# Attention inputs laid out by channel: no transposes in, one scan for the states, 96-column sums on TensorE

## The reference, cut to what matters

```python
for t in range(S):                                   # S = 768
    kt, vt, rt, wt = (k[:, :, t], v[:, :, t], r[:, :, t], w[:, :, t])
    cur = np.einsum('bhd,bhe->bhde', u[None] * kt, vt)
    y[:, :, t] = np.einsum('bhd,bhde->bhe', rt, state + cur)
    state = wt[:, :, :, None] * state + np.einsum('bhd,bhe->bhde', kt, vt)
x = _moe_ref(x=x, **moe_kwargs)      # dense: every token through 8 experts
return _moe2_ref(x=x, **moe2_kwargs) # routed: every token through one expert
```

## Time and profile before

| | |
|---|---|
| time, median of 3 runs | 1204.25 us (1198.97 to 1204.97) |
| time of the profiled execution | 1201.32 us |
| its span | 1199.6 us |
| PE busy in the span | 97% |
| DVE, ACT, POOL busy | 42%, 37%, 20% |
| last instruction of the attention ends | 150.34 us |
| mean granted clock of TensorE, whole span | 0.978 |
| mean granted clock, 25.30 to 138.60 us | 0.80 |

### The profile page before, as it was taken

How to read it: one execution, slowest core, us unless ns; L and a number is a source line. 1 busy time by engine, 2 the same in 40 slices (tenths; PEclk the granted TensorE clock), 3 DMA queues, 4 the chain that set the end, 5 groups by cost and what they waited for, 6 DMA issues and landing times. The chain is left out here.

```text
span 1199.6 us, 18556 instructions
## 1 busy us (share of the span) xinstructions
PE 1161.1 (97%) x6968; PEld 1039.6 (87%) x6968; DVE 504.4 (42%) x949; ACT 448.9 (37%) x926; POOL 243.8 (20%) x247
## 2 busy tenths in 40 slices
PE   6999989999999999999999999999999998999997
PEld 4888769899999998999999899999999986999997
DVE  5777556222222222212222222212222353999996
ACT  4565352212212211221221122122123473888884
POOL 5544262202201210220221121022012210000001
PEclk9888799999999999999999999999999999999999
DMA  9741043040050031005005002200300303999991
GB/s 187 144 70 31 2 149 124 26 160 1 1 186 1 1 132 55 1 2 185 1 1 185 1 1 91 94 1 1 105 1 1 132 35 114 392 358 368 359 361 59
DMA packets 106982, 123.41 MB, mean 103 GB/s; under 512 B 52745, under 2 KB 95406, under 8 KB 106912
## 3 DMA queue, kind: packets, MB, share of 16 engines
q1 hardware_dynamic: 104928, 117.65, 31.1%
q0 software_dynamic: 1984, 4.75, 1.0%
HBM read 98.37 MB, written 25.39 MB: 103 GB/s over the span
## 5 line engine op out<-in xcount | busy, mean ns | idle before, releaser
L973 DVE SCALAR_TENSOR_TENSOR h_lo<-hid,h_hi 128x512 fp32r<-128x512 f32 x168 | 116.1, 691 | 497.8 <-ACT h_hi L836 497.8
L836 ACT ACTIVATE h_hi<-hid 128x512 fp32r<-128x512 f32 x168 | 100.5, 598 | 547.7 <-PE hid L1131 547.7
L794 POOL TENSOR_TENSOR w_lo<-raw,w_hi 128x384 fp32r<-128x384 f32 x128 | 130.8, 1022 | 644.2 <-ACT w_hi L828 644.2
L1144 PE MATMUL acc<-w_hi,h_hi 128*128 128x384 f32 x736 | 249.6, 339 | 0.0
L1144 PE MATMUL acc<-w_hi,h_lo 128*128 128x384 f32 x736 | 249.3, 339 | 0.0
L1144 PE MATMUL acc<-w_lo,h_hi 128*128 128x384 f32 x736 | 248.6, 338 | 0.0
L1131 PE MATMUL hid<-x_hi,w_hi 128*128 128x512 f32 x576 | 227.9, 396 | 0.5 <-issue 0.4
L1131 PE MATMUL hid<-x_hi,w_lo 128*128 128x512 f32 x576 | 227.6, 395 | 0.0
L1131 PE MATMUL hid<-x_lo,w_hi 128*128 128x512 f32 x576 | 227.3, 395 | 0.0
L1144 PEld LDWEIGHTS acc<-w_lo,h_hi 128*128 128x128 f32 x736 | 138.1, 188 | 8.6
L1144 PEld LDWEIGHTS acc<-w_hi,h_hi 128*128 128x128 f32 x736 | 138.1, 188 | 7.7
(11 more groups left out here) (255 smaller groups left out, 1464.1 us busy)
## 6 DMA issues: line engine op xcount, KB each, us to landing
raw<-in_moe_w SPq DMA_DIRECT2D x54, 1536.0 KB, 9.2
rows<-filler SPq DMA_DIRECT2D x8, 2328.0 KB, 16.4
m_x<-rows SPq DMA_DIRECT2D x19, 194.0 KB, 4.6
spread_w<-in_w SPq DMA_DIRECT2D x16, 144.0 KB, 4.2
spread_r<-in_r SPq DMA_DIRECT2D x16, 144.0 KB, 4.1
spread_k<-in_k SPq DMA_DIRECT2D x16, 144.0 KB, 4.3
v_sb<-in_v SPq DMA_DIRECT2D x16, 144.0 KB, 4.2
out_y<-m_y,m_token POOLq DMA_INDIRECT x19, 6.7
```

Of the source, the lines that this page charges most:

```text
L794: pool.tensor_tensor(lo[q][m][:, a:b], raw[m][:, a:b], hi[q][m][:, a:b].bitcast(F32), ALU.subtract).then_inc(s_wlo, 1)
L836: act.activation(h_hi[st % HB][:, :], hid[st % HB][:, :], ACT.Relu).then_inc(s_hhi, 1)
L973: dve.scalar_tensor_tensor(h_lo[st % HB][:, :], hid[st % HB][:, :], 0.0, h_hi[st % HB][:, :].bitcast(F32), ALU.max, ALU.subtract).then_inc ...
L1144: mm = pe.matmul(acc[j][:, 0:DM], a[st % HB][:, j * P:(j + 1) * P], b[q][1][:, f * DM:(f + 1) * DM], start=(f == 0 and x == 0), stop=(f == ...
```

## The change

The host lays the inputs out before the launch. `laid_out` gives r and k by channel, with 64 rows for each head and zeros in rows 48 to 63, w in the same way with ones there and with the scan's zeros between the blocks, v by token and padded to one run per partition, and u as 96 columns for each pair of heads, of which two hold u and the other 94 are zero. So each of a pair's inputs is one DMA, straight into `w_pad`, `k_ch`, `r_ch` and `v_sb`, and `turn_in`, `channels`, the `spread` tensors and their memsets go.

The u term is now one POOL multiplication of 768 columns (`rk`), six PE matmuls of 96 columns (`sums`), and a copy of 12 columns on ACT (`current`). The states are one DVE scan over 240 columns with a table `carry`, which ACT fills (`carries`). Scores have four PSUM banks in place of two. On DVE both scans of the next pair are ahead of the states of this one. `keep_clock` has one matmul of 240 columns for each pair, where it had three of 256 (`FIRST, BACK, LAST = 5, 1, 4`: five ahead of the first pair, one for each later pair, four at the end).

```diff
@@ sync
-                for n in "wrk":
-                    for h in two:
-                        sp.dma_start(spread[n][q][:, :, h, 0:D], src[n][i, h]).then_inc(s_in[n][q], 16)
+                load(w_pad, w, "w", i)
+                load(k_ch, k, "k", i)
+                load(r_ch, r, "r", i)
@@ gpsimd
-                pool.tensor_tensor(rku[:, :, :, :], spread["r"][q][:, :, :, 0:D], spread["k"][q][:, :, :, 0:D], ALU.mult).then_inc(s_rk, 1)
-                pool.tensor_tensor(rku[:, :, :, :].rearrange("p n h d -> p n (h d)"), rku[:, :, :, :].rearrange("p n h d -> p n (h d)"),
-                                   u_rows[:, c:c + 2 * D].unsqueeze(1).broadcast_to([P, NT, 2 * D]), ALU.mult).then_inc(s_rku, 1)
+                if j >= 1:
+                    pool.wait_ge(s_sums, j)
+                pool.tensor_tensor(rk[:, :], r_ch[j % 2][:, :], k_ch[j % 2][:, :], ALU.mult).then_inc(s_rk, 1)
+            receiver_keys(0)
+            for j in range(PAIRS):
+                scaled(j)
+                if j + 1 < PAIRS:
+                    receiver_keys(j + 1)
+                current_values(j)
@@ scalar
-                act.activation(block_w[q][:, :, 1:BLK1], turn_a[:, 0:S].rearrange("p (n c) -> p n c", c=BLK), ACT.Copy).then_inc(s_chan["w"], 1)
-                act.activation(r_ch[q][:, :], turn_b[:, 0:S], ACT.Copy).then_inc(s_chan["r"], 1)
-                act.activation(k_ch[q][:, :], turn_a[:, 0:S], ACT.Copy).then_inc(s_chan["k"], 1)
+            def carries(j):
...
+                act.activation(carry[j % 2][:, :, 1:NT - 1], coef_r[:, 1:NT - 1, BT].unsqueeze(1).broadcast_to([P, D, NT - 2]),
+                               ACT.Copy).then_inc(s_carry, 1)
+            def current(j):
+                act.wait_ge(s_sums, j + 1)
...
+                act.activation(flat(cur[j % 2][:, :, :]), turn[:, CUR:CUR + NT * 2], ACT.Copy).then_inc(s_cur, 1)
+            current(0)
+            for j in range(PAIRS):
+                divided(j, 0)
+                carries(j)
+                rows(j)
+                halves(j)
+                divided(j, 1)
+                diagonal(j)
+                if j + 1 < PAIRS:
+                    current(j + 1)
@@ vector
-                dve.tensor_copy(st[:, 1, :], inc[:, 0, :]).then_inc(s_step, 1)
-                for t in range(1, NT - 1):
-                    dve.wait_ge(s_step, (NT - 2) * i + t)
-                    step = dve.scalar_tensor_tensor(st[:, t + 1, :], st[:, t, :], coef_r[:, t, BT:BT + 1], inc[:, t, :], ALU.mult, ALU.add)
-                dve.tensor_reduce(cur[:, :, :], rku[:, :, :, :], AX.X, ALU.add).then_inc(s_cur, 1)
+                dve.tensor_tensor_scan(state[q][:, :, :].rearrange("p d t -> p (d t)"), carry[q][:, :, :].rearrange("p d t -> p (d t)"),
+                                       turn[:, 0:(NT - 1) * D], 0.0, ALU.mult, ALU.add).then_inc(s_state, 1)
             for i in range(-1, PAIRS):
+                if ahead:
+                    before_block(i + 1)
+                if ahead:
+                    behind_block(i + 1)
                 if back:
                     states(i)
-                if ahead:
-                    before_block(i + 1)
+                if i >= 1:
+                    outputs(i - 1, 1)
@@ tensor
+            def sums(j):
+                pe.wait_ge(s_rk, j + 1)
+                for t in range(NT):
+                    mm = pe.matmul(turn[:, CUR + 2 * t:CUR + 2 * t + WIDE], rk[:, t * P:(t + 1) * P], u_cols[:, j % (H // 2), :],
+                                   start=True, stop=True, skip_group_check=True)
+                mm.then_inc(s_sums, 1)
+            for j in range(PAIRS):
+                pe.wait_ge(s_cur, j + 1)
+                keep_clock(FIRST if j == 0 else BACK)
+                turn_back(j)
+                if j >= 1:
+                    out_tiles(j - 1, 1)
+                increments(j)
+                scores(j, 0)
+                if j + 1 < PAIRS:
+                    sums(j + 1)
+                scores(j, 1)
+                out_tiles(j, 0)
```

More of the change, by code:

```diff
@@ L89, in attention @@
         k_rows = sb("k_rows", [P, NT, P])
[L90 removed]
+        state = [sb(f"state{q}", [P, D, NT - 1]) for q in two]
         state_diag = [sb(f"state_diag{q}", [P, NT, 2, 64]) for q in two]
[L92 to L93 removed]
+        carry = [sb(f"carry{q}", [P, D, NT - 1]) for q in two]
+        rk = sb("rk", [P, S])
+        cur = [sb(f"cur{q}", [P, NT, 2]) for q in two]
         cur_v = sb("cur_v", [P, NT, 2, D])
         scores_sb = [[sb(f"scores_sb{g}{h}", [P, TG, P]) for h in two] for g in range(G)]
[L97 to L99 removed]
+        turn = ps("turn", [P, 1024])
+        CUR, IDLE = S, S + 16
+        score = [[ps(f"score{g}{h}", [P, 512]) for h in two] for g in range(G)]
         yps = [ps(f"yps{g}", [P, 512]) for g in range(G)]
@@ L297, in _ @@
             dve.memset(tile_end[:, :, BT:BT1], 1.0).then_inc(s_link, 1)
-            for q in two:
-                diag = dve.memset(state_diag[q][:, :, :, :], 0.0)
-            diag.then_inc(d_init, 1)
             done = [4]
@@ L1705, with laid_out @@
 _INS = ["r", "k", "v", "w", "u", "moe_w_gate", "moe_w1", "moe_w2", "moe2_expert_emb", "moe2_tau", "moe2_w1", "moe2_w2"]
+def laid_out(name, a):
+    a = np.atleast_1d(a)
+    if name in ("r", "k"):
+        rows = np.zeros((PAIRS, 2, 64, S), a.dtype)
+        rows[:, :, :D] = a.reshape(PAIRS, 2, S, D).transpose(0, 1, 3, 2)
+        a = rows.reshape(PAIRS, P, S)
+    if name == "w":
+        w = np.ones((PAIRS, 2, 64, NB * (BLK + 1) + 1), a.dtype)
+        w[..., ::BLK + 1] = 0
+        w[:, :, :D, :-1].reshape(PAIRS, 2, D, NB, BLK + 1)[..., 1:] = a.reshape(PAIRS, 2, NB, BLK, D).transpose(0, 1, 4, 2, 3)
+        a = w.reshape(PAIRS, P, -1)
+    if name == "v":
+        a = a.reshape(PAIRS, 2, NT, P, D).transpose(0, 3, 1, 2, 4).reshape(PAIRS, P, 2 * NT * D)
+    if name == "u":
+        u = np.zeros((2, 64, H // 2, WIDE), a.dtype)
+        for h in range(2):
+            u[h, :D, :, h] = a[h::2].T
+        a = u.reshape(P, H // 2, WIDE)
+    return np.ascontiguousarray(a)
 def kernel(**inputs):
@@ L1714 @@
     for name in _INS:
-        a = np.atleast_1d(np.ascontiguousarray(inputs[name]))
+        a = laid_out(name, inputs[name])
         arrays[f"in_{name}"] = a
```

231 lines of the change are left out of this document (78 added, 153 removed).

## The result

The changed kernel takes 1188.31 us (median of 11 runs, 1185.48 to 1193.13). The kernel before, run beside it on the same chip, took 1198.97 (11 runs, 1195.24 to 1204.97). The medians differ by 10.7 us and the means by 11.7. The ratio over all runs is 0.9903, 95% interval 0.9879 to 0.9926: the change is 1.0% faster. The forecast was 1189.5 us. A part of that closeness is luck: the forecast started from the median of three runs, 1204.25, which the later runs put 5 us lower. From 1198.97 the same sum gives 1184.4, 3.9 us under what was measured. Execution against execution, the profiled one was forecast at 1186.7 us and took 1190.21, against 1201.32 before; so 14.6 us were forecast and 11.1 came.

What follows compares the result with a forecast made beforehand. PE was taken to set the period, through its clock. Start 22.4, seven periods 103.6 and end 9.7 make 135.7 instead of 150.34 us; 1204.25 - 14.6 = 1189.6, say 1189.5 us, range 1175 to 1204.

Steps and rivals of the forecast that it cites:

- What bounds the kernel, and the rest behind the attention: PE sets the attention's period, at a mean clock of 0.80; the 1049.2 us stretch behind the attention is left alone.
- The period at full clock, 12.9 us: Loop from `receivers` through POOL, DVE and PE: 12.9 us, above PE's own 10.9, so PE waits 2 us for `rk`.
- the estimate of 1.6 us: POOL's `rk` by about 2.5 cycles an element at 1.2 GHz; the prediction took 1.8 us instead.
- The period at the low clock, 18.9 us: PE's own list at the low level takes 18.9 us, is the longer one and hides POOL.
- The mix: Both periods weighted by the old clock shares, 60% high and 40% low: 14.8 us a period, 103.6 us for seven.
- The start, 22.4 us: First states at 22.4 us instead of 25.30, with PE's four matmuls of 384 columns at 3.5 us.
- The end, 9.7 us: From the last states to the last `x_tok`: scores, outputs and four `keep_clock`, 9.7 us instead of 11.8.
- The high clock throughout: Rival: the sums fill the gap between the scores, period 12.9 us throughout, 1176.3 us; chance 0.15.
- the low clock: Rival: PE loses its densest work and the clock stays low; slower from a 75% low share, 1214 to 1225 us; chance 0.11.
- POOL taking back most of the gain: Rival: DVE and POOL take turns, gaps of 3 us make the period 16 us, 1198 us; chance 0.15.

Runs made afterwards that it cites:

- values_on_act: combined2 with the values times cur (`cur_v`) moved from one POOL instruction to 12 small ones on ACT; 1163.28 us, 0.9696 of the kernel before.
- rk_sooner_back2: Changed kernel with POOL's `rk` between the halves and `r_tile`, and two `keep_clock` matmuls a pair instead of one; 1168.61 us, 0.9746 of the kernel before.
- back3: Changed kernel with three `keep_clock` matmuls of 240 columns ahead of each `turn_back` instead of one; 1176.15 us, 0.9803 of the kernel before.
- rk_sooner: Changed kernel with POOL's `rk` of the next pair between the halves and `r_tile`, not behind `r_tile`; 1176.60 us, 0.9799 of the kernel before.
- start_sooner: Changed kernel with the first pair's sums ahead of PE's four 384-column matmuls and without the five first `keep_clock` matmuls; 1185.99 us, 0.9891 of the kernel before.
- combined2: rk_sooner_back2 and start_sooner together, against the changed kernel; 1168.67 us, 0.9739 of the kernel before.
- rk_twice: Changed kernel with POOL's multiplication `rk` issued twice in each pair, same values; 1196.32 us, 0.9982 of the kernel before.
- chain: Changed kernel with the states' one scan undone: a copy and four multiply-adds of 48 columns, as before the change; 1187.84 us, 0.9895 of the kernel before.
- sooner_narrow: rk_sooner with the six sums matmuls streaming 2 columns in place of 96; 1195.59 us, 0.9965 of the kernel before.

## Why the prediction was right, and where it was off

**What bounds the kernel, and the rest behind the attention.** Right: 1048.5 us follow the last output in place of 1049.2.

**The period at full clock, 12.9 us.** Right, and for the reason given: between PE's own marks it is 12.56 and 12.71 us, with 11.04 of work (10.9 forecast) and a wait for `rk` of 1.53 and 1.67 (2 forecast). From the end of `receivers` to the end of `rk` it is 7.1 us, where the terms add up to 7.6. `rk` takes 1.81 us (1.8) and the sums 1.5 (1.35). The rule of the Trainium skill's "SBUF — State Buffer", section "Who interferes with whom", agrees again: 2.98 us for `r_tile` and 3.30 for `rk`, which take 1.48 and 1.81 alone, and values_on_act gained 0.5 us a period by taking one of POOL's reads out. For `rk`, the estimate of 1.6 us by the Trainium skill's "GPSIMD Engine Reference" (the C++ chunk loop) was low. The 12.4 to 12.9 us of rk_sooner_back2 are another loop, DVE's and POOL's with a wait for `k_tile`.

**The period at the low clock, 18.9 us.** Right: 19.24 us twice, with PE never waiting. The sums took 2.88 us (2.6).

**The mix.** This is the step that was mis-sized: "Mixed in the shares of before (60% and 40% of the time)". The low clock held for 57% of the seven periods, and the seven took 106.7 us and not 103.6: 3.1 of the 4.3 us by which the end was late. By the prediction's own formula a share of 57% makes a period of 15.75 us and seven of them 110.3. That it was less is a second error, which lay the other way: the prediction counted seven equal periods, but the last one prepares no further pair and took 10.15 us. At full clock throughout, rk_sooner_back2's seven take 85.0 us and not 90.3. So the number was helped by luck here too.

The share is no constant of the kernel but an outcome of the list, and even for one list it varies from execution to execution: the 40% come from one execution, with a mean clock of 0.978, while others of the kernel before had 0.972 to 0.989. Before's six low stretches last 3.4 to 13.7 us, the two of after 30.7 each. That this comes from the dense matmuls that went is what back3 speaks for, with one stretch of 13.7 us and 0.93; that the late `rk` starts them, rk_sooner, with 0.89. Both edits together hold the clock at 1.00, and without the 96 columns it is at 0.67 even with no wait. The prediction had named both facts, as the reasons against one rival and for another, and then took the old share all the same. The price of the low clock can be checked: 61.4 us at 19.24 us a period are 3.2 periods, which at 12.4 take 39.7. That makes 21.7 us, and the seven periods of rk_sooner_back2 are 21.8 us shorter.

**The start, 22.4 us.** 1.3 late: the four matmuls of 384 columns took 5.49 us and not 3.5. I had scaled the two of before, taken to run as the clock rose. The durations of the start look like the low level: the first sums of start_sooner take 2.88 us, as at 0.50. But the granted clock that the profile gives is 1.00 from the start of the span, for both kernels, so "the clock rising", and "at the low clock" in the expectation of start_sooner, are not shown by it. start_sooner shows a second thing that the sum left out: ACT's `k_div` stood behind the copy of the first sums, until 18.9.

**The end, 9.7 us.** From the last states at 130.46 to 140.05 it is 9.6.

**The rivals.** The high clock throughout came only in the variants. It was priced too high, by the same seven equal periods: rk_sooner_back2, combined2 and values_on_act have the clock at 1.00 and take 1168.6, 1168.7 and 1163.3 us, not 1176.3. That rk_sooner and back3 measured 1176.6 and 1176.2 is chance, for both had a low stretch. The reason against this rival, that PE waits longer for `rk` than it did for `k_rows` and such waits came ahead of the drops, was the right one. For the low clock, the share stayed under the 75% from which it would have been slower. POOL taking back most of the gain did not come in the change. rk_twice lost the gain, but by the low clock (0.67) and not by longer fast periods, which stayed at 12.7 us.

What stays open: why a wait of 1.53 us leaves the clock up in chain and not in the change, and what in PE's list sets the length of a low stretch. The runs only rank lists of instructions.

## What to carry to other kernels

When a change takes dense work from a TensorE list that already swings between two clocks, don't price it with the old share: read which matmuls stand around each drop, and take a range from the fast period to the slow one. Don't take a full busy share of TensorE as a sign of a high clock; read the granted clock. Columns of zeros beside the useful ones can be a cheap cure: here they took 0.08 to 0.15 us a pair. Where another engine's instruction is waited for by TensorE, put it ahead of its neighbours that nobody waits for before buying anything else: here one moved line gave as much again as the whole change.

## What the hardware showed that was not expected

TensorE was busy in 107.7 of 107.7 us in sooner_narrow and had a mean clock of 0.67, while it was busy for 80.7 of 85.0 us in combined2 and had 1.00. So busy time alone did not keep the clock up in the one, and five waits of up to 0.9 us did not bring it down in the other. The six matmuls that differ between sooner_narrow and rk_sooner take nearly the same time in the trace with 2 columns as with 96. And both low stretches of the change were 30.7 us long, with PE busy in all but 0.2 us of them, before the clock rose again.
